# Attention, sparse experts and a feed-forward block on one core: the value products of one query block in one group

## The reference

```python
batch, n_heads, seq, head_dim = (2, 8, 768, 64)
n_sink, window = (4, 128)
...
scores = scale * np.matmul(q, k.transpose(0, 1, 3, 2))
is_sink = pos[None, :] < int(n_sink)
rel = pos[:, None] - pos[None, :]
in_window = (rel >= 0) & (rel < int(window))
keep = is_sink | in_window
scores = np.where(keep, scores, -1000000000.0)
scores = scores - np.max(scores, axis=-1, keepdims=True)
a = np.exp(scores)
a = a / (np.sum(a, axis=-1, keepdims=True) + 1e-09)
return np.matmul(a, v).astype(np.float32)
...
x = attn_out.transpose(0, 2, 1, 3).reshape(B * S, H * D)
x = _moe_ref(x=x, **moe_kwargs)      # 8 experts of 192 tokens: relu(x @ w1[e]) @ w2[e]
return _moe2_ref(x=x, **moe2_kwargs) # h = x @ w_in; (max(h, 0) + alpha * min(h, 0)) @ w_out
```

## Time and profile before

| | |
|---|---|
| median of 3 runs | 638.41 us (637.21 to 638.51) |
| the profiled execution | 638.79 us |
| its span, first to last instruction | 637.0 us |
| TensorE busy | 620.3 us (97%) |
| VectorE, ScalarE, GpSimd busy | 419.9, 308.3, 196.5 us |
| granted TensorE clock, mean | 0.99 |

### The profile page before, as it was taken

One profiled execution on the slowest core, in us unless ns is written; L12 is line 12 of the kernel. 1 busy time (PEld: TensorE's weight loads), 2 busy tenths in 40 slices (PEclk: granted clock), 3 DMA queues, 4 the chain that ended last, 5 costly groups with the idle time before them and its releaser, 6 DMA issues.

```text
span 637.0 us, 12935 instructions
## 1 busy us (share of the span) xinstructions
PE 620.3 (97%) x4949; PEld 557.9 (88%) x4954; DVE 419.9 (66%) x1156; ACT 308.3 (48%) x716; POOL 196.5 (31%) x211
## 2 busy tenths in 40 slices
PE   8899999899999999999999999999999999999996
PEld 4789998759899888899999888999989989999995
DVE  7788887978576979844759798438587520035552
ACT  5888884511132655532236554322465642346663
POOL 4998881010111342111113431211233410113331
PEclk9899999889999999999999999999999999999999
DMA  7477854535450143037002510370016610000001
GB/s 260 150 256 274 273 192 157 191 94 198 139 203 1 67 158 116 2 104 253 35 2 85 206 51 2 117 273 1 2 67 227 243 75 17 1 1 1 1 1 50
DMA packets 31221, 72.37 MB, mean 114 GB/s; under 512 B 2876, under 2 KB 2936, under 8 KB 31160
## 3 DMA queue, kind: packets, MB, share of 16 engines
q1 hardware_dynamic: 27232, 60.69, 27.2%
q0 software_dynamic: 1984, 6.29, 2.9%
q10 hardware_dynamic: 1944, 4.56, 2.0%
HBM read 65.22 MB, written 6.32 MB: 112 GB/s over the span
## 4 chain that ended last, share of the span: by engine, by line
PE 76%; DVE 3%; DMA 1%; issue 0%; POOLq 0%; POOL 0%; ACT 0%
PE bank L1602 21%; PE bank L1617 21%; PE bank L1514 14%; PE bank L1505 13%; PE bank L1392 3%; DVE beats L971 1%; DMA rank_row<-key_row 1%; PE bank L1483 1%; PE bank L1461 1%; DVE beats L942 1%; PE bank L1233 1%; PE bank L1445 0%; PE bank L1438 0%; PE bank L1394 0%; DVE ties L984 0%
## 5 line engine op out<-in xcount | busy, mean ns | idle before, releaser
L603 POOL TENSOR_TENSOR wi_lo<-w_in,wi_hi 128x512 fp32r<-128x512 f32 x64 | 89.2, 1396 | 274.4 <-ACT wi_hi L744 274.4
L942 DVE TENSOR_SCALAR beats<-rank_row,key 128x512 bf16<-128x512 f32 (+11 forms) x144 | 92.3, 661 | 12.4 <-PE bank L1394 12.4
L1617 PE MATMUL bank<-wo_lo,g_hi 128*128 128x512 f32 x192 | 76.0, 396 | 0.0
L1617 PE MATMUL bank<-wo_hi,g_lo 128*128 128x512 f32 x192 | 75.7, 394 | 0.0
L1617 PE MATMUL bank<-wo_hi,g_hi 128*128 128x512 f32 x192 | 75.5, 393 | 0.0
L1215 DVE SCALAR_TENSOR_TENSOR g<-bank,g_neg 128x384 f32<-128x384 f32 x64 | 35.5, 554 | 52.9 <-ACT g_neg L796 52.9
L794 ACT ACTIVATE g_neg<-bank 128x384 f32<-128x384 f32 x64 | 31.4, 491 | 79.9 <-PE bank L1602 79.1
L1602 PE MATMUL bank<-y_hi,wi_hi 128*128 128x384 f32 x256 | 57.8, 347 | 0.0
L770 ACT ACTIVATE h_t<-bank 128x192 f32<-128x192 f32 x64 | 21.1, 330 | 74.2 <-PE bank L1505 71.3
L670 ACT ACTIVATE prob<-neg_s,neg_max 128x260 f32<-128x260 f32 x96 | 48.9, 510 | 15.4 <-DVE neg_max L853 13.2
L1602 PE MATMUL bank<-y_lo,wi_hi 128*128 128x384 f32 x256 | 55.2, 336 | 0.0
(11 more groups left out here) (180 smaller groups left out, 1369.3 us busy)
## 6 DMA issues: line engine op xcount, KB each, us to landing
w_a<-moe_w SPq DMA_DIRECT2D x8, 1024.0 KB, 5.2
w_a<-moe_w SPq DMA_DIRECT2D x4, 2048.0 KB, 11.3
w_b<-moe_w SPq DMA_DIRECT2D x8, 1024.0 KB, 5.2
w_b<-moe_w SPq DMA_DIRECT2D x4, 2048.0 KB, 10.2
k_raw<-k_t SPq DMA_DIRECT2D x11, 512.0 KB, 4.8
q_raw<-q_t SPq DMA_DIRECT2D x11, 512.0 KB, 3.9
w_in<-moe_w_in SPq DMA_DIRECT2D x8, 512.0 KB, 5.0
w_out<-moe_w_out SPq DMA_DIRECT2D x8, 512.0 KB, 4.7
```

Of the source, the lines that this page charges most:

```text
L603: nc.gpsimd.tensor_tensor(out=wi_lo[:, f % 2, :, :], in0=w_in[:, :, f * P:(f + 1) * P], in1=wi_hi[:, f % 2, :, :].bitcast(F32), op=ALU.sub ...
L942: return nc.vector.tensor_scalar(out=beats[:, c % 3, lo:hi], in0=rank_row[:, lo:hi], scalar1=key[:, c:c + 1], scalar2=None, op0=op)
L1617: last = nc.tensor.matmul(DOWN_BANK[t][:, :], a[:, f % 3, t * P:(t + 1) * P], w[:, f % 2, :], start=(f == 0 and n == 0), stop=(f == FC - 1 ...
```

## The change

On TensorE the value products of pairs 0 and 1 of a step leave the end of the slot that turns it (behind head 7) and go behind head 1 of the next slot, directly ahead of those of pairs 2 and 3. On VectorE the copy of pair 0 goes from behind the maximum of head 1 to behind that of head 2, and the sums with their reciprocal from head 2 to head 1. The numbering of the copies stays as it is. Nothing is computed otherwise.

```diff
--- before.py
+++ after.py
@@ -877,7 +877,7 @@
                                                 axis=AX, op=ALU.add).then_inc(x_ready, 1)
                     if 0 <= mid < STEPS:
                         b, i = step(mid)
-                        if h == 2:
+                        if h == 1:
                             dve.wait_ge(exped, H * (mid + 1))
                             chain.after(nc.vector.tensor_reduce(out=p_add[:, :], in_=p_sum[b][:, :, :], axis=AX, op=ALU.add))
                             nc.vector.reciprocal(p_inv[b][:, :], p_add[:, :]).then_inc(sums_read, 1)
@@ -885,8 +885,8 @@
                             dve.wait_ge(st_copied, mid + 1)
                             nc.vector.tensor_tensor(out=sink_t[SR:2 * SR, :], in0=SINKS[SR:2 * SR, :],
                                                     in1=sink_t[SR:2 * SR, :].bitcast(F32), op=ALU.subtract).then_inc(st_split, 1)
-                        if h in (1, 5, 7):
-                            g = 4 * mid + h // 2
+                        if h in (2, 5, 7):
+                            g = 4 * mid + (0 if h == 2 else h // 2)
                             dve.wait_ge(pt_done, g + 1)
                             if g >= PAIRS:
                                 dve.wait_ge(pv_done, g - PAIRS + 1)
@@ -1345,8 +1345,8 @@
                     elif front < STEPS:
                         keep_clock(5 if h == H // 2 - 1 else 1, OT_BANK)
                     if h == 1 and 0 <= end < STEPS:
-                        values(end, 2)
-                        values(end, 3)
+                        for r in range(PAIRS):
+                            values(end, r)
                     if h == sinks_at(mid) and 0 <= mid < STEPS:
                         turn_sinks(mid)
                     if h == 4 and 0 <= end < STEPS:
@@ -1355,9 +1355,6 @@
                         sink_values(mid)
                     if h == 6 and 0 <= end < STEPS:
                         turn_and_gate(end, 0)
-                    if h == 7 and 0 <= mid < STEPS:
-                        values(mid, 0)
-                        values(mid, 1)
 
             pe.wait_ge(zeros_ready, 1)
             keep_clock(19, PT_BANK[0])
```

## The result

The changed kernel takes 641.61 us (median of 10 runs, 639.44 to 644.09), the kernel before 638.46 in the same comparison (10 runs, 637.21 to 639.25). The ratio is 1.0048, with an interval of 1.0037 to 1.0059: slower, by 3.15 us. The profiled execution took 641.37. Among the executions used in this document one, of the kernel before on the chip of e1 to e4, took 865.74 us at a mean granted clock of 0.65 and is left out of the ratios.

The account below looks back on a forecast made before the run. TensorE was taken to set the pace in attention, at 7.62 us a slot. Slots 4 to 11 at +0.09 each (+0.72) and slot 12 (+0.88) gave +1.60 on 638.41, so 640.0; range 637.8 to 641.8.

Parts of the forecast that it names:

- rival 3: GpSimd overtakes if VectorE's second half slips another 0.3: slot 7.85, +2.7, 641.1 us; decides past 7.83; chance 0.15.
- The merge saves 0.34 per slot: TensorE's value products: a separate group costs 1.22, two more pairs in a standing group 0.88, so each merge saves 0.34.
- The copy comes too late for the turn of head 4: VectorE's copy of pair 0 ends at 4.66 in the slot; TensorE's turn, due at 4.25, must wait for it.
- The price of that wait, 0.43: TensorE's turn of head 4 waits 0.47, less a little regained, so 0.43 per slot; bounds 0 and 0.55.
- GpSimd has become as long as TensorE: GpSimd's round of two slots becomes 15.39, one slot not under 7.70, adding nothing to TensorE's 7.71.
- my signs of being wrong: Turns of head 4 without wait, slots 7.5 or less, or head 0's scores waiting over 0.1 for GpSimd.
- Slots 2 and 3 go into GpSimd's waits: GpSimd sets the starts of slots 2 to 4, so changes in slots 1 to 3 vanish in waits, costing 0.
- rival 4: Clock or the serial part behind attention shifts; a low stretch met or missed may be worth 1 us either way; chance 0.10.
- Slot 12 costs 0.88 and gives nothing back: Slot 12, without scores behind it, receives 0.88 of value products; its gate product waits for the output copy, so +0.88.
- Rival 1: The wait at head 4's turn does not bite: slots 7.5 through GpSimd, -0.4, 638.0 us; chance 0.15.
- Rival 2: All saved TensorE gaps count: 8 x -0.34 + 0.88 = -1.8, 636.6 us; chance 0.05.
- Rival 5: The merge saves nothing because gaps remain inside TensorE's group; held excluded by the group of 32, no chance given.

Follow-up runs that it names:

- e1: Changed kernel with VectorE's old order back, so TensorE's merge of the value products alone; 638.27 us, ratio 0.9998 to the kernel before.
- e4: e1 with GpSimd rounding the next q ahead of packing the sinks; 637.29 us, ratio 0.9981 to the kernel before.
- e3: Changed kernel plus four matmuls of zeros at the end of slot 1 to keep TensorE busy; 640.33 us, ratio 1.0034 to the kernel before.
- e11: The changed kernel itself, measured again on the chip of e9; 641.27 us, ratio 1.0039 to the kernel before.
- e9: Changed kernel plus ten matmuls of zeros in slot 1, behind heads 5, 6 and 7; 639.90 us, ratio 1.0027 to the kernel before.
- e2: Kernel before with VectorE's half of the change alone (later copy of pair 0, earlier sums); 642.16 us, ratio 1.0055 to the kernel before.
- e8: e3 with GpSimd rounding the next q ahead of packing the sinks; 641.06 us, ratio 1.0036 to the kernel before.
- e7: e1 plus four matmuls of zeros at the end of slot 1; 637.17 us, ratio 0.9978 to the kernel before.
- e5: e4 plus four matmuls of zeros at the end of slot 1; 636.89 us, ratio 0.9974 to the kernel before.
- e6: Kernel before with only the first block's products of pairs 0 and 1 moved from slot 1 to slot 2; 639.35 us, ratio 1.0011.

## Why the prediction came out as it did

The direction was right and the time lay in the range, but the loss is 3.15 where I forecast 1.60. That it lay in the range is partly luck: the forecast's own part ended at +2.6, and the range was drawn on to 641.8 for rival 3, whose mechanism did not come about. What the named mechanism costs can be read from the three profiles in which the changed kernel, with or without zeros, kept its clock in slot 2: from slot 2 to the keys e3, e11 and e9 take 2.11, 2.12 and 2.18 more than the kernel before. Of the 0.5 to 0.6 above 1.60 nearly all is the wait's price, mis-sized. In the first profile it was +3.34, and the further 1.2 goes with the low clock. Step by step:

- **The merge saves 0.34 per slot.** Right. In e1 a slot that nothing holds takes 7.27, in the kernel before 7.61.
- **The copy comes too late for the turn of head 4.** Right in place and mechanism: the copy was to end 4.66 into the slot and ended at 69.77 - 65.10 = 4.67. e1 and e2 show it by taking it out and by putting it in alone.
- **The price of that wait, 0.43.** Mis-sized. I took 0.05 from VectorE's release to the load, after a row in which GpSimd released TensorE; from VectorE's copy it is 0.11 in both kernels that wait, close to the 0.12 that I had as the upper bound from the earlier trace rows (with 0.12 that sum gives 0.53, not the 0.55 that I wrote). With it the wait costs 0.49 to 0.50 and a slot is 7.77, not 7.71. Over seven slots that is 0.42 of the 0.61 missing in the third row of the table.
- **GpSimd has become as long as TensorE.** Right in size. The last maximum starts 72.96 - 65.10 = 7.86 into the slot (I had 7.80), which with 7.59 makes a round of two slots 15.45, or 7.73 each, just under 7.77. That is past the 7.83 at which rival 3 was to decide, but this figure belonged to a slot of 7.71; for one of 7.77 it is 7.95. e8, in which GpSimd has room, has the same slots.
- **The other 0.20 of the third row** is the start of slot 6, behind the second mask, 0.16 late for GpSimd. By the letter this is one of my signs of being wrong (GpSimd named with more than 0.1). It came in that profile only: in e3, e9 and e11 GpSimd holds slot 4 for 0.50 to 0.52 and slot 6 not at all, and the seven slots take 54.33 to 54.41, not 54.54. I put it down to the low clock, which had made slot 4 start late: GpSimd's packing ahead of the second mask began 1.23 into slot 4, and 0.68 into it in e11. No run shows this by itself.
- **Slots 2 and 3 go into GpSimd's waits.** Right where the clock holds (16.13 in e3 and e11, against 16.11), wrong in the profile of the changed kernel. I had the clock as rival 4, but at the 0.47 wait of each slot and behind attention. I wrote that the 1.22 leaving slot 1 goes into a wait and costs nothing, and did not ask what that idle time does to TensorE. The waits of 0.48 in each slot did not lower the clock: it was 1.00 from 34 to 104 us in the changed kernel's profile.
- **Slot 12 costs 0.88 and gives nothing back.** Right: slot 11 and what follows cost 1.07 where 0.09 + 0.88 + the mis-sized 0.06 make 1.03.
- **Rival 1** (the wait gone, slots of 7.5, -0.4) is e1: mean slots of 7.48, and a time of -0.1; its profile has the low clock in slot 2. With the filling, e7, it is -1.0. **Rival 2** is not to be had without touching GpSimd; e4 and e5 get -1.1 and -1.2. **Rival 3** did not come about, though its 641.1 is nearer to the measured time than my 640.0. **Rival 4**, to which I gave 0.10, is the best reading of what came on top, at a place where I had not looked. **Rival 5** fell with the group of 32.

## What to carry to other kernels

A step moved behind another engine's result inherits that result's lateness: price it from the row that it now stands behind, add the release (0.11 us here from a copy to a weight load), and compare with the place of whoever waits for it. When an edit takes work out of a stretch where TensorE waits anyway, look at the gap that it leaves: here the wait grew from 0.64 to 1.55 us, and the clock was low behind it in all five profiles with such a gap, though it isn't shown that the gap is the cause. And where one engine's gain is small, work out the next engine's round first: here GpSimd's round took 0.21 of a gain of 0.34 per slot, and a change of order in its list, with no work removed, gave it back.

## What the runs showed of the hardware

A release from VectorE's copy to TensorE's weight load takes 0.11 us (changed kernel and e2), from GpSimd's subtraction 0.04 to 0.06; I had expected one figure for both. And the same program meets its low clock in different places: at 24 to 28 us in the changed kernel's first profile, at 16 to 20 us in e11. The kernel before has it at 16 to 21 us, and e9 nowhere from 14 to 34 us. In slot 1 it costs nothing (10.31 and 10.32 with it, 10.31 in e2 without). In slot 2 it goes with 1.03 us more for slots 2 and 3 in the changed kernel, and with 2.84 more in e6. The runs of the changed kernel spread over 4.7 us and, in e11, over 4.2, where those of the kernel before spread over 2.0 to 3.3 in the four comparisons; the low clock is the likely reason, but no run shows that.
